# Block sums of V by adding DMAs issued by GpSimd, in place of loads in fours and VectorE additions

## The reference

```python
B, H, S, D = 4, 8, 576, 64; factor = 4; Sd = S // factor
q_d = q.reshape(B, H, Sd, factor, D).mean(axis=3)
k_d = k.reshape(B, H, Sd, factor, D).mean(axis=3)
v_d = v.reshape(B, H, Sd, factor, D).mean(axis=3)
out_d = sm_attn(q_d, k_d, v_d)
out_up = np.repeat(out_d, factor, axis=2)
...   # out_local: full-resolution attention where |i - j| < factor
return (out_up + out_local)
```

## Time and profile before

| what | value |
|---|---|
| median of 3 runs | 978.68 us (975.21 to 984.75) |
| profiled execution | 975.69 us |
| its span, first to last instruction | 973.9 us |
| mean granted TensorE clock in it | 0.965 |
| busy: PE, DVE, ACT, POOL | 939.7, 657.6, 432.9, 592.6 us |
| bytes moved by DMA | 63.93 MB |

### The profile page before, as it was taken

The page is one execution under the profiler, slowest core; times in us unless marked ns, Lnnn a source line. Parts: engine busy times, 40 slices in busy tenths (PEclk is TensorE's granted clock), DMA queues, the critical chain, the costliest instruction groups (busy, mean ns, idle before and its releaser), DMA issues.

```text
span 973.9 us, 17619 instructions
## 1 busy us (share of the span) xinstructions
PE 939.7 (96%) x6056; PEld 846.1 (87%) x6056; DVE 657.6 (68%) x978; ACT 432.9 (44%) x1029; POOL 592.6 (61%) x627
## 2 busy tenths in 40 slices
PE   6999988999999999999999999999999999999998
PEld 5677766899998999999999998999898989899896
DVE  6689795668888578877555687667774456744453
ACT  3567455544445644445444455333442324332221
POOL 2386576887788768878676775455644445543520
PEclk9689776999999999999999999999999999999999
DMA  9878200322211111121111122121103011030101
GB/s 236 158 179 221 56 1 18 109 66 65 66 44 44 44 44 45 44 66 42 47 44 45 44 87 71 60 77 54 44 22 108 23 43 39 28 109 22 44 1 65
DMA packets 57556, 63.93 MB, mean 66 GB/s; under 512 B 5500, under 2 KB 50428, under 8 KB 57084
## 3 DMA queue, kind: packets, MB, share of 16 engines
q1 hardware_dynamic: 55884, 61.63, 22.3%
q10 hardware_dynamic: 1584, 1.18, 0.4%
HBM read 58.07 MB, written 4.72 MB: 64 GB/s over the span
## 4 chain that ended last, share of the span: by engine, by line
PE 83%; DVE 7%; issue 4%; POOL 3%; ACT 2%; DMA 1%; SPq 1%; ACTq 0%; DVEq 0%; POOLq 0%
PE bank L1365 43%; PE bank L1420 20%; PE bank L1395 14%; DVE xs L1013 1%; PE bank L1283 1%; PE bank L1323 1%; PE bank L1298 1%; PE bank L1277 1%; POOL prob L511 1%; PE bank L1302 1%; ACT xs L686 1%; DMA stage<-w_dram 1%; DMA kp<-k_dram 1%; POOL xcomb L562 1%; DVE mxl L870 1%
## 5 line engine op out<-in xcount | busy, mean ns | idle before, releaser
L1365 PE MATMUL bank<-xs,wst 128*128 128x384 f32 x2520 | 503.1, 339 | 5.1 <-DVE vt L1082 2.8
L1365 PEld LDWEIGHTS bank<-xs,wst 128*128 128x128 f32 x2520 | 441.5, 188 | 29.3 <-issue 10.2
L550 POOL TENSOR_TENSOR wst<-wraw,wst 128x256 fp32r<-128x256 f32 x240 | 230.6, 979 | 141.0 <-ACT wst L651 139.5
L1420 PE MATMUL bank<-wo,gs 128*128 128x512 f32 x864 | 218.4, 393 | 1.4 <-ACT xT L760 0.8
L1395 PE MATMUL bank<-hb,wo 128*128 128x512 f32 x864 | 189.0, 336 | 1.3 <-DVE hb L1092 1.3
L1420 PEld LDWEIGHTS bank<-wo,gs 128*128 128x128 f32 x864 | 160.4, 188 | 29.8 <-DVE gs L1113 1.1
L1395 PEld LDWEIGHTS bank<-hb,wo 128*128 128x128 f32 x864 | 146.0, 188 | 9.9 <-issue 1.6
L1082 DVE TENSOR_TENSOR vt<-u,bank 128x384 f32<-128x384 f32 x120 | 66.2, 552 | 122.6 <-PE bank L1365 122.6
L651 ACT CAST wst<-wraw 128x256 fp32r<-128x256 f32 x360 | 122.9, 407 | 0.0
L533 POOL TENSOR_TENSOR wraw<-wraw,stage 128x256 f32<-128x256 f32 x60 | 51.0, 849 | 93.2 <-DMA wraw<-w_dram 93.1
L736 ACT ACTIVATE sig<-gt 128x384 f32<-128x384 f32 x72 | 37.9, 526 | 125.7 <-DVE gt L1082 124.5
(11 more groups left out here) (102 smaller groups left out, 1065.7 us busy)
## 6 DMA issues: line engine op xcount, KB each, us to landing
wraw<-w_dram SPq DMA_DIRECT2D x180, 128.0 KB, 2.3
stage<-w_dram SPq DMA_DIRECT2D x60, 128.0 KB, 2.1
woraw<-w_dram SPq DMA_DIRECT2D x28, 256.0 KB, 3.5
vquad<-v_dram SPq DMA_DIRECT2D x16, 288.0 KB
out_dram<-xT SPq DMA_DIRECT2D x18, 256.0 KB, 2.9
kp<-k_dram SPq DMA_DIRECT2D x3, 1152.0 KB, 8.7
qs<-q_dram SPq DMA_DIRECT2D x3, 1152.0 KB, 14.4
vwin<-v_dram SPq DMA_DIRECT2D x6, 512.0 KB
```

Of the source, the lines that this page charges most:

```text
L550: nc.gpsimd.tensor_tensor(b[:, 1, :], w_source(w, p), b[:, 0, :].bitcast(fp32), ALU.subtract).then_inc(wlp_done, 1)
L1365: last = mm(XY[s % 2][:, 0:HC], wst[:, u % 2, p, pw, 128 * k:128 * k + 128], xs[:, p, px, k, :], start=(p not in CONTINUES and i == 0 and ...
L1420: last = mm(ACC[t][:, :], gs[:, v % 2, m, px, 128 * t:128 * t + 128], wo[:, 2 * j + m, pw, :], start=(j == 0 and n < 18 and i == 0), stop= ...
```

## The change

The three DVE additions, the tile vquad and its loads go. vd gets two slots, for even and odd groups. For each group SP loads the first of every four rows straight into vd (`load_first_values`, two DMAs of 144 KB, waiting for the value products of group b - 2), and POOL issues for each of the other three two DMAs that add the rows of V to what lies in vd (`add_values`). POOL does that after the normalise of steps i = 6, 8 and 10 in group 0 and i = 1, 4 and 9 in the others, and waits each time until the DMAs before have landed. PE waits for the last of them.

```diff
-SUM_V_AT = (10, 11, 12)
+ADD_V_AT = (1, 4, 9)
+FIRST_ADD_V_AT = (6, 8, 10)
...
-        vquad = sb("vquad", [HK, 2, 2, FACTOR, GC], stack=att)
-        vd = sb("vd", [HK, 2, 2, GC], stack=att)
+        vd = sb("vd", [HK, 2, 2, 2, GC], stack=att)
...
+        def values_of(b, x, r):
+            v = v_d[batch0(b) + x][:, D * head0(b):D * head0(b) + GC]
+            return v.rearrange("(k p r) n -> p r k n", k=2, r=FACTOR)[:, r]
...
-            def load_vquad(b):
-                ready(sp, vd_done, 3 * b)
+            def load_first_values(b):
+                ready(sp, pv_done, NU * (b - 1))
                 for x in range(2):
-                    for kt in range(2):
-                        v = v_d[batch0(b) + x][S // 2 * kt:S // 2 * kt + S // 2, D * head0(b):D * head0(b) + GC]
-                        sp.dma_start(vquad[:, kt, x, :, :],
-                                     v.rearrange("(p r) n -> p r n", r=FACTOR)).then_inc(vq_in, 16)
+                    sp.dma_start(vd[:, b % 2, :, x, :], values_of(b, x, 0)).then_inc(vd_in[b][0], 16)
...
+            def add_values(b, r):
+                for x in range(2):
+                    if x == 0:
+                        pool.wait_ge(vd_in[b][r - 1], 32)
+                    nc.gpsimd.dma_start(vd[:, b % 2, :, x, :], values_of(b, x, r),
+                                        accum_op=ALU.add).then_inc(vd_in[b][r], 16)
...
+                add_at = FIRST_ADD_V_AT if b == 0 else ADD_V_AT
+                if i in add_at:
+                    add_values(b, add_at.index(i) + 1)
...
-                if i in SUM_V_AT:
-                    sum_values(b, SUM_V_AT.index(i))
...
                     if p == 0 and x == 0:
-                        pe.wait_ge(vd_done, 3 * (b + 1))
+                        pe.wait_ge(vd_in[b][FACTOR - 1], 32)
```

More of the change, by code:

```diff
@@ L229, in fused_kernel @@
         v_part = [sem("v_part0"), sem("v_part1")]
-        vq_in = sem("vq_in")
         misc_in = sem("misc_in")
@@ L248, in fused_kernel @@
         ks_done = sem("ks_done")
-        vd_done = sem("vd_done")
+        vd_in = [[sem(f"vd_in{b}_{r}") for r in range(FACTOR)] for b in range(NG)]
         x_done = sem("x_done")
@@ L442, in _ @@
             load_v(0, V_PARTS[1], V_PARTS[2], v_in[0])
-            load_vquad(0)
+            load_first_values(0)
             for b in range(1, NG):
@@ L455, in _ @@
                 load_v(b, 0, NL, v_in[b])
-                load_vquad(b)
+                load_first_values(b)
                 if b == 1:
@@ L913, in sum_four @@
                 nc.vector.reduce_sum(dst, src.rearrange("p a (s r) -> p a s r", r=FACTOR), AX).then_inc(ks_done, 1)
[L915 to L924, removed]
             def sum_squares(q, k):
@@ L1333, in values @@
                             c = D * (2 * p + h)
-                            last = mm(output_bank(g)[halves[h], 0:SD], vd[:, kt, x, c:c + D],
+                            last = mm(output_bank(g)[halves[h], 0:SD], vd[:, b % 2, kt, x, c:c + D],
                                       pdT[:, n % 2, kt, :, h, :], start=(kt == 0), stop=(kt == 1))
```

## The result

| what | before | after |
|---|---|---|
| median | 978.84 us (975.21 to 984.75) | 1008.1 us (1007.65 to 1011.45) |
| span of the profiled execution | 973.9 us | 1006.6 us |
| mean granted TensorE clock | 0.965 | 0.946 |
| first product of the feed-forward layers begins | 160.06 us | 191.62 us |

The ratio is 1.0291, interval 1.0254 to 1.0328. The change costs 29 us, and the forecast of 979 and its range to 993 missed it.

A forecast was written before the change was run, and what follows sets the result against it. PE alone bounds the kernel from 400 us; the change acts in the attention stage, where PE, DVE, ACT and POOL alternate. Terms 2.5 + 1.3 + 0.4 - 1.1 + 0.3 = +3.4 on 975.7 gave 979 us, range 970 to 993.

The forecast's parts named there:

- L: Time from the issue of a pair of POOL's DMAs to its landing: between 2.1 and 9.2 us, taken as 5.5.
- 23.18 + 3 I + 3 L: Group 0: when vd is complete, three chained pairs behind the normalise of unit 5 ending at 23.18; predicted 46.3 us.
- I: Time in which POOL issues a pair of DMAs: between 0.54 and 4.4 us, taken as 2.2.
- The +2.5 at V(9): Group 0: PE's value products of unit 9, first to read vd, wait for its last pair; +2.5 us.
- rival 1: Slower: pairs land late, seen at POOL's waits at steps 8 and 10 and at V(9); 990 to 995 us, chance 0.22.
- So the normalises stay covered: late is vd: Group 0: third pair holds POOL until 40.0, ahead of PE's transposes of unit 10, T(10), at 42.8; no PE wait for normalises.
- +1.3 and +0.4: Group 1: pair of step 17 costs +1.3 us at PE's transposes of unit 21, T(21); pair of step 22 costs +0.4.
- Step 30: Group 2: its pair fits into the 2.6 us POOL no longer waits ahead of line 533; no cost.
- SP's release, -1.1: Group 2: SP, not waiting for DVE's last add, sends the weight load some 4 us earlier; PE gains 1.1 us.
- The clock: Attention stage: a shifted wait can lose or spare a half-clock stretch of PE, some 5 us either way; no mean.
- rival 3's gains: Cheap issue and landing leave only gains: -1.0 at unit 21's normalise, -1.1 at T(28), -1.4 in group 3; 972 us, chance 0.11.

The follow-up runs named there:

- the run with SP held: Changed kernel with pairs of groups 1 to 3 at steps 0, 3, 5, and SP holding K, Q, V of groups 2 and 3 until the previous third pair landed: 988.31 us.
- the run with no chain and more space: Changed kernel with second and third pairs adding into tiles of their own, unchained, and descriptor space 1792 instead of 1024; sums incomplete: 997.14 us.
- both remedies: Changed kernel with group 0 back to fours and DVE's adds, groups 1 to 3 with pairs at steps 0, 3, 5 and SP's loads held: 983.97 us.
- The two runs with one part each: Changed kernel with group 0 back to fours and DVE's adds, 1000.78 us; changed kernel with pairs in group 0 only, the others in fours, 1002.45 us.

## Why the prediction was wrong

- **The term that failed: L.** "L is between 2.1 and 9.2, and I take 5.5, nearer to the plain row." Measured in group 0 it was 11.5, 8.7 and 6.3, mean 8.8, close to the upper bound and for the first pair beyond it. The formula was right: 23.18 + 3 I + 3 L with I = 2.3 and L = 8.8 gives 56.5, and vd was complete at 56.98. The +2.5 at V(9) should have been +13.3. The row that showed such a delay was K of group 1 with 16.0 us; the prediction quoted it for rival 1 and against the page's fit, but sized its own term by ACT's 4.4.
- **Its reason.** The doubling for the addition, the prediction's argument for more than 4.6, is the smaller part: alone, a DMA of a pair takes 4.0 to 4.8 us with it and 2.9 without, beside the loads in group 0 6.6 to 12.2 with it and 8.5 to 10.6 without. What makes L is SP's queue. Rival 1 names this mechanism and its place, steps 8 and 10 and V(9), and even K of group 2; the run with SP held shows it for the second and third pair. It had a chance of 0.22, and its price ended at 995.
- **L is not all.** With L = 8.8 rival 1's own prices (3L - 14.05 at V(9), L - 4.7 at step 17, and 0.9) make 17.4 us, about 993; measured were 31.6 at the first product. Some 14 us lie outside the term: 4.0 between V(9) (+13.3) and unit 16 (+17.3), where nothing waits and V(9) takes 1.23 us instead of 0.71, so at half clock; 6.3 at step 30 (below); and 8.2 from unit 34 to the first product, where no landing holds POOL and whose cause no run isolates. Step 17's share of 4.1 didn't come at all.
- **Group 0's normalises.** "So the normalises stay covered: late is vd" failed with it: POOL was held 8.99 us at step 8, and T(8) waited 7.08. The reading had a slip as well: by its own terms, 23.18 + 3 I + 2 L, the third pair holds POOL until 40.8, not 40.0. Nothing hung on that.
- **Group 1, +1.3 and +0.4.** Partly there, by another way. Step 17 waited for no landing, but behind its pair (71.71) POOL is busy without a gap, and PE waits for a normalise at T(17) to T(21), 0.26 to 0.48 us each and 1.7 together. The qk products go from 17.3 us late at unit 16 to 18.5 at unit 24, and back to 16.8 at unit 25, behind T(21), whose wait of 1.33 is now 0.33. Where group 0 is on time, step 17 waits 5.67 for its landing: there the term was missized by the same L.
- **Step 30**, "lies in the 2.6 us that POOL gets back". The line 533 wait did go, but the pair of step 27 (96.53) fell beside K, Q and V of group 3, which SP issued from 93.06; POOL waited 3.60 and T(30) 5.29. PE's delay goes from 17.1 at unit 33 to 23.4 at unit 34.
- **SP's release, -1.1.** Right by itself (-1.2 at unit 32), and given back before the stage ended.
- **I.** 2.30 us a pair against the 2.2 taken, 1.15 for each DMA.
- **The clock**, "I put no mean on it". In the profiled executions half clock rose from 69 to 109 us, and PE's own work took 10.0 us longer, a third of the loss; a price of zero was the second error. The rest is idle time of PE: the four in the rows above, 7.08, 4.16, 3.92 and 5.29, are 20.5 of the 22.7 us that PE idles more. Yet no rule of so much clock for so much waiting comes out: the run with no chain and more space idles longest, 59.1 us with one wait of 12.98, and its PE is busy for 935.0, less than before; the one with both remedies hardly waits and has 947.8. (Part of that is the single execution: the 935.0 come from a run at 0.964, and the other three of that kernel had 0.951 to 0.960.)
- **What was removed** was worth more than the 3.5 us of rival 3's gains: 9 us in time without the pairs.

What stays open: how the 31.6 us divide among the three stops, and why the clock fell as it did. The two runs with one part each don't add up; as their rows read, each late group moves the next one's pairs to another place in SP's loads, and to another clock.

## What to carry to other kernels

Price a DMA by what else is on the engines in the time of its flight, from a row of a transfer in that same time, and never from one that had less beside it; a chain of small dependent DMAs pays that price at each link. Don't put a wait for a landing on an engine that others wait for in order: the wait costs every instruction behind it. Where PE swings between two clocks, a saved or added wait of a few microseconds doesn't arrive at the end as such, so a change that is only meant to unload DVE should be tried without its replacement first, to see what it can bring at all.

## What the runs showed of the hardware

- GpSimd stops at the issue of a DMA, with no semaphore and no releaser in the profile, while earlier DMAs of it have not drained: 8.45 and 7.55 us with pairs of 2 x 144 KB and a declared space of 1024, none and 4.70 with 1792. With half the size the second pair went out while the first was still in flight, and the one stop in group 0 was 1.41.
- A pair of adding DMAs of 144 rows of 1 KB keeps POOL for 2.3 us, a plain one for 1.4; alone each DMA lands in 4.0 to 4.8 and in 2.9 us. The adding pair made 416 packets and kept the sixteen engines for 34.2% of 6 us, so 2.1 us of all of them; the plain one made 128 packets and took 11.0% of 8 us, 0.9.
- Beside K, Q and V on SP's queue the size of POOL's DMAs counted little: 72 KB took 11.1 and 8.8 us to their landing in the first two pairs, 144 KB 11.9 and 9.5.
- The Trainium skill (DMA: Bandwidth & Descriptors, Anatomy of one DMA — SWDGE (gpsimd) path) has a fit that the prediction worked out as 2.3 us. The plain and lone DMA is 0.6 above it; with the addition, or beside another queue's loads (6.6 to 12.2), it doesn't hold.
- The remedied version idles as little as before and is yet slower, by 8.1 us more of PE's busy time for the same 6056 matmuls. The kernel before, with nothing changed, took 974.02 us at a mean clock of 0.968 and 983.89 at 0.951: on this kernel a difference in clock goes with up to 1% of the time, so it can hide or undo a change of half a per cent.
